# Attention and two MLP layers in float32: a new instruction order over 16 blocks, and weight preparation moved into attention

## What is computed

```python
# attention: 12288 queries, kv (384, 32, 128) pooled 4x4 to 768 keys
kv_pool = kv.reshape(B, H // r, r, W // r, r, C).mean(axis=(2, 4))
k = v = kv_pool.reshape(B, -1, C) @ w_sr
s = scale * (q @ k.transpose(0, 2, 1)); s = s - s.max(-1, keepdims=True)
a = np.exp(s); a /= a.sum(-1, keepdims=True) + 1e-09
x = a @ v
# layer 1
h = x @ w_in
x = (np.maximum(h, 0.0) + alpha * np.minimum(h, 0.0)) @ w_out
# layer 2
h = x @ w_in2; h2 = h * h; h3 = h2 * h
P = a[0] + a[1] * h + a[2] * h2 + a[3] * h3
Q = 1.0 + np.abs(b[0]) * np.abs(h) + np.abs(b[1]) * h2
out = (P / (Q + 1e-06)) @ w_out2
```

## Time and profile before

| | us |
|---|---|
| median of 3 runs (lowest, highest) | 1619.42 (1613.58, 1620.19) |
| the profiled execution's own time | 1616.42 |
| its span, first to last instruction | 1614.3 |

### The profile page before, as it was taken

How to read it: one execution, slowest core, us unless ns; L and a number is a source line. 1 busy time by engine, 2 the same in 40 slices (tenths; PEclk the granted TensorE clock), 3 DMA queues, 4 the chain that set the end, 5 groups by cost and what they waited for, 6 DMA issues and landing times. The chain is left out here.

```text
span 1614.3 us, 22125 instructions
## 1 busy us (share of the span) xinstructions
PE 1555.7 (96%) x5869; PEld 1015.0 (63%) x5869; DVE 1412.7 (88%) x2175; ACT 1398.8 (87%) x2659; POOL 1149.2 (71%) x1256
## 2 busy tenths in 40 slices
PE   6899999989999999999999999999999999999976
PEld 5799999845566565655565555656656555656532
DVE  3688888727999999999999999999999999999997
ACT  2577777628999999999999999999999999999996
POOL 0344444306888888888888888888888888888887
PEclk9999999999999999999999999999999999999998
DMA  8110100000000000000000000000000000000000
...
DMA packets 12299, 24.54 MB, mean 15 GB/s; under 512 B 1536, under 2 KB 1680, under 8 KB 11920
## 3 DMA queue, kind: packets, MB, share of 16 engines
...
q10 hardware_dynamic: 752, 0.60, 0.1%
...
## 5 line engine op out<-in xcount | busy, mean ns | idle before, releaser
L256 POOL TENSOR_TENSOR cubic<-sq,lin_p 128x512 f32<-128x512 f32 x384 | 492.4, 1283 | 225.4 <-ACT lin_p L408 178.0
L659 PE MATMUL banks<-x_hi,win_lo 128*128 128x512 f32 x768 | 508.4, 662 | 25.2 <-DVE ratio L591 15.3
L248 POOL TENSOR_TENSOR rational<-newton,ratio 128x512 f32<-128x512 f32 x288 | 368.6, 1280 | 35.8 <-PE banks L829 13.6
L818 PE MATMUL banks<-neg_part,wout 128*128 128x512 f32 x768 | 388.0, 593 | 0.3 <-ACT neg_part L386 0.3
L829 PE MATMUL banks<-rational,wout 128*128 128x512 f32 x768 | 379.2, 601 | 4.2 <-POOL rational L248 4.1
L577 DVE SCALAR_TENSOR_TENSOR banks<-sq,abs_b,banks 128x512 f32<-128x512 f32 x384 | 282.3, 752 | 59.2 <-ACT banks L402 57.2
L661 PE MATMUL banks<-x_hi,win_hi 128*128 128x512 f32 x768 | 303.7, 395 | 0.0
L660 PE MATMUL banks<-x_lo,win_hi 128*128 128x512 f32 x768 | 303.3, 395 | 0.0
L591 DVE SCALAR_TENSOR_TENSOR ratio<-banks,ab_raw,rcp 128x512 f32<-128x512 f32 x384 | 285.5, 743 | 1.3 <-ACT rcp L422 1.2
L583 DVE SCALAR_TENSOR_TENSOR banks<-banks,ab_raw,cubic 128x512 f32<-128x512 f32 x384 | 280.0, 752 | 0.0
L659 PEld LDWEIGHTS banks<-x_hi,win_lo 128*128 128x128 f32 x768 | 145.1, 189 | 205.1 <-issue 67.7
...
## 6 DMA issues: line engine op xcount, KB each, us to landing
...
```

The source lines that it names most:

```text
L248: nc.gpsimd.tensor_tensor(rational[:, m % 3, :], newton[:, m % 2, :], ratio[:, m % 2, :], ALU.mult).then_inc(s["rat_done"], 1)
L256: nc.gpsimd.tensor_tensor(cubic[:, m % 2, :], sq[:, m % 2, :], lin_p[:, m % 2, :], ALU.mult).then_inc(s["cubic_done"], 1)
L659: nc.tensor.matmul(dst, w[1], x[0], start=start, stop=False)
L818: nc.tensor.matmul(banks[:, ACC1, :], wout1[:, c, :], neg_part[:, n % 2, :], start=False, stop=(c == BLOCKS - 1)).then_inc(s["m1_done"], 1)
```

## The change

Layers: the pattern of four blocks gives way to one order of 16 blocks, written out for each engine, with layer 2 following 18 blocks behind. The win1 parts are negated, so that the negative part is a plain Relu. For the eight odd blocks the negative part is split (`neg_hi` by ScalarE, `neg_lo` by VectorE) and `out1` makes three float32r passes with a split w_out1. Of the others VectorE makes the negative part of block 14 alone; it keeps the finals of blocks 4 and 12 instead of four. `out2` makes four products of 128 columns with the data as weights, so that ACC2 comes out with the tokens in the partitions; the copy and the transposes of the output are gone. `negative` waits for `m1_done` of n - 3 instead of n - 1.

Load and attention: kv is loaded first. w_in1 is turned in step 0, the linear weight made in step 1, w_in1 split in steps 4 to 7 and w_in2 in steps 10 to 13 in pieces of 512 columns, w_out1 scaled in steps 16 to 19. The queries of group g + 1 are turned in step g, those of group 1 in the load phase. After the last step w_out1's odd blocks are split, and TensorE's first hidden product waits for that.

The diff, cut to its core:

```diff
-QUAD = 4
-DEPTH = 5 * QUAD
-BY_DVE_FINAL, BY_DVE_RELU = 2, 3
+BY_DVE_FINAL, BY_DVE_RELU = (4, 12), (14,)
+SPLIT = (1, 3, 5, 7, 9, 11, 13, 15)
...
+        wout1_hi, wout1_lo = sb("wout1_hi", [P, len(SPLIT), P], F32R), sb("wout1_lo", [P, len(SPLIT), P], F32R)
+        neg_hi, neg_lo = sb("neg_hi", [P, 2, GROUP], F32R), sb("neg_lo", [P, 2, GROUP], F32R)
...
+        IN1_STEP, IN2_STEP, SCALE_STEP, OUT2_STEP = 4, 10, 16, 15
+        PIECES = 4
...
-            sp.dma_start(raw_in[0], w_in1).then_inc(s["ld_in1"], 16)
             for c in range(CHUNKS):
-                if c == 3:
-                    sp.dma_start(wout1[:], w_out1.rearrange("(b p) c -> p b c", p=P)).then_inc(s["ld_out1"], 16)
-            sp.wait_ge(s["v_lo_done"], 2)
-            sp.dma_start(raw_in[1], w_in2).then_inc(s["ld_in2"], 16)
-            with sp.Fori(0, GROUPS // 2 - 1) as pair:
-                for u in (0, 1):
-                    sp.wait_ge(s["qt_ready"], pair * 2 + (1 + u))
-                    sp.dma_start(q_in[:, u, :], q_groups[pair * 2 + (2 + u)]).then_inc(s[f"ld_q{u}"], 16)
-
-            sp.wait_ge(s["in2_lo_done"], 1)
-            sp.dma_start(wout2[:], w_out2.rearrange("(b p) c -> p b c", p=P)).then_inc(s["ld_out2"], 16)
+            sp.dma_start(raw_in[0], w_in1).then_inc(s["ld_in1"], 16)
+            sp.dma_start(wout1[:], w_out1.rearrange("(b p) c -> p b c", p=P)).then_inc(s["ld_out1"], 16)
+            for g in range(GROUPS - 2):
+                sp.wait_ge(s["qt_ready"], g + 1)
+                sp.dma_start(q_in[:, g % 2, :], q_groups[g + 2]).then_inc(s[f"ld_q{g % 2}"], 16)
+                if g == 2:
+                    sp.wait_ge(s["v_lo_done"], 2)
+                    sp.dma_start(raw_in[1], w_in2).then_inc(s["ld_in2"], 16)
+                if g == OUT2_STEP:
+                    sp.wait_ge(s["in2_lo_done"], PIECES)
+                    sp.dma_start(wout2[:], w_out2.rearrange("(b p) c -> p b c", p=P)).then_inc(s["ld_out2"], 16)
             with sp.Fori(0, GROUPS) as g:
...
         @block.gpsimd
...
+            for p in range(GROUPS + 2):
+                final(p - 2, 14)
+                correction(p - 2, 15)
+                cubic_term(p - 1, 1)
+                final(p - 2, 15)
...
+                correction(p - 1, 14)
+                cubic_term(p, 0)
 
...
         @block.scalar
...
+                nc.scalar.activation(hi[:, piece(k)], raw[:, piece(k)], ACT.Copy, scale=-1.0 if name == "in1" else 1.0).then_inc(s[f"{name}_hi_done"], 1)
 
             act.wait_ge(s["ld_ab"], 32)
...
-            in1_transposed()
             copy_pooled_t(0)
             query_hi(0)
-            weight_hi(raw_in[0], win1_hi, "in1")
             copy_pooled_t(1)
-            act.wait_ge(s["lin_ready"], 1)
-            nc.scalar.activation(lin_hi[:], banks[:, 1, 0:P], ACT.Copy).then_inc(s["lin_hi_done"], 1)
+            query_hi(1)
             copy_pooled_t(2)
             copy_pooled_t(3)
...
                 exps(g, 0)
                 probs_hi(g - 2, 5)
                 exps(g, 1)
+                if g == 0:
+                    in1_transposed(0)
+                    in1_transposed(1)
+                if g == 1:
+                    linear_hi()
                 probs_hi(g - 1, 0)
                 attended_hi(g - 2)
                 probs_hi(g - 1, 1)
                 exps(g, 2)
-            weight_hi(raw_in[1], win2_hi, "in2")
+                if g == 0:
+                    in1_transposed(2)
+                    in1_transposed(3)
+                if IN1_STEP <= g < IN1_STEP + PIECES:
+                    weight_hi(raw_in[0], win1_hi, "in1", g - IN1_STEP)
+                if IN2_STEP <= g < IN2_STEP + PIECES:
+                    weight_hi(raw_in[1], win2_hi, "in2", g - IN2_STEP)
+            act.wait_ge(s["out1_scaled"], PIECES)
+            act.wait_ge(s["s_ready"], GROUPS * TILES)
+            nc.scalar.activation(wout1_hi[:], wout1_odd, ACT.Copy).then_inc(s["out1_hi_done"], 1)
 
 
...
+                    after(act, s["m1_done"], n - 3)
+                    kept = neg_hi if c in SPLIT else neg_part
+                    nc.scalar.activation(kept[:, c // 2 % 2, :], banks[:, H1, :], ACT.Relu).then_inc(s["neg_done"], 1)
...
+            for p in range(GROUPS + 3):
+                scaled_abs(p - 3, 14)
+                hidden_hi(p - 2)
+                square(p - 3, 15)
+                scaled_abs(p - 3, 15)
+                linear_part(p - 3, 15)
+                log(p - 3, 14)
+                negative(p - 1, 1)
+                inverse_q(p - 3, 14)
+                log(p - 3, 15)
+                linear_part(p - 2, 0)
+                square(p - 2, 0)
+                inverse_q(p - 3, 15)
+                scaled_abs(p - 2, 0)
+                negative(p - 1, 2)
...
+                inverse_q(p - 2, 13)
+                negative(p, 0)
...
         @block.vector
...
                 dve.wait_ge(s[f"ld_{name}"], 16)
-                dve.wait_ge(s[f"{name}_hi_done"], 1)
-                nc.vector.tensor_tensor(lo[:], raw, hi[:].bitcast(F32), ALU.subtract).then_inc(s[f"{name}_lo_done"], 1)
+                dve.wait_ge(s[f"{name}_hi_done"], k + 1)
+                nc.vector.scalar_tensor_tensor(lo[:, piece(k)], raw[:, piece(k)], -1.0 if name == "in1" else 1.0,
+                                               hi[:, piece(k)].bitcast(F32), ALU.mult, ALU.subtract).then_inc(s[f"{name}_lo_done"], 1)
...
+            def scale_out1(k):
...
-            weight_lo(raw_in[0], win1_hi, win1_lo, "in1")
+            query_lo(1)
             pool_keys(3)
-            dve.wait_ge(s["lin_hi_done"], 1)
-            nc.vector.tensor_tensor(lin_lo[:], banks[:, 1, 0:P], lin_hi[:].bitcast(F32),
-                                    ALU.subtract).then_inc(s["lin_lo_done"], 1)
             pool_keys(4)
             keys_lo(0)
             pool_keys(5)
+            values_lo(0)
             keys_lo(1)
-            values_lo(0)
-            values_lo(1)
             for g in range(STEPS):
                 if g > 0:
-                    query_lo(g)
+                    query_lo(g + 1)
                 probs_lo(g - 2, 2)
...
+                if SCALE_STEP <= g < SCALE_STEP + PIECES:
+                    scale_out1(g - SCALE_STEP)
+            dve.wait_ge(s["out1_hi_done"], 1)
+            nc.vector.tensor_tensor(wout1_lo[:], wout1_odd, wout1_hi[:].bitcast(F32), ALU.subtract).then_inc(s["out1_lo_done"], 1)
...
+            def negative_lo(g, c):
+                if group(g):
+                    dve.wait_ge(s["neg_done"], made(g, c, BY_ACT_RELU))
+                    nc.vector.scalar_tensor_tensor(neg_lo[:, c // 2 % 2, :], banks[:, H1, :], 0.0,
+                                                   neg_hi[:, c // 2 % 2, :].bitcast(F32),
+                                                   ALU.max, ALU.subtract).then_inc(s["neg_lo_done"], 1)
...
+                    nc.vector.tensor_scalar(y_out[:], banks[:, ACC2, :], -1.0, None, ALU.mult).then_inc(s["y2_out_done"], 1)
...
+            for p in range(GROUPS + 3):
+                place_output(p - 3)
+                denominator(p - 2, 3)
+                polynomial(p - 2, 2)
+                negative_lo(p - 1, 5)
+                check_product(p - 2, 2)
+                quotient(p - 2, 2)
+                check_product(p - 2, 3)
+                polynomial(p - 2, 3)
+                denominator(p - 2, 4)
+                quotient(p - 2, 3)
+                denominator(p - 2, 5)
+                polynomial(p - 2, 4)
+                negative_lo(p - 1, 7)
+                quotient(p - 2, 4)
+                check_product(p - 2, 4)
...
         @block.tensor
...
+            def linear_weight(first, end):
...
             pe.wait_ge(s["k_lo_done"], 2)
-            pe.wait_ge(s["v_lo_done"], 2)
             for g in range(STEPS):
                 if g > 0:
-                    queries(g)
+                    queries(g + 1)
                 weighted(g - 2, 0)
                 weighted(g - 2, 1)
                 transposed(g - 2, 3)
                 tile_scores(g, 0)
+                if g == 1:
+                    linear_weight(0, 6)
                 transposed(g - 2, 4)
                 weighted(g - 2, 2)
                 tile_scores(g, 1)
+                if g == 0:
+                    turn_in1(0)
+                    turn_in1(1)
+                if g == 1:
+                    linear_weight(6, 11)
                 weighted(g - 2, 3)
                 transposed(g - 2, 5)
                 weighted(g - 2, 4)
                 tile_scores(g, 2)
+                if g == 1:
+                    linear_weight(11, BLOCKS)
                 transposed(g - 1, 0)
                 weighted(g - 2, 5)
                 transposed(g - 1, 1)
                 tile_scores(g, 3)
+                if g == 0:
+                    turn_in1(2)
+                    turn_in1(3)
                 transposed(g - 1, 2)
 
 
-            for name in ("in1_lo_done", "lin_lo_done", "out1_scaled"):
-                pe.wait_ge(s[name], 1)
```

(65 more changed lines are left out.)

583 lines of the change are left out of this document (355 added, 228 removed).

## The result

| | before | after |
|---|---|---|
| median of the runs | 1618.54 us (4 runs, 1613.58 to 1620.19) | 1562.49 us (4 runs, 1560.67 to 1564.52) |
| ratio, 95% interval | | 0.9659 [0.9634, 0.9684] |
| profiled execution, its span | 1616.4, 1614.3 | 1564.5, 1562.7 |

A forecast was written before the change was run, and what follows sets the result against it. TensorE was taken to bound the kernel before and after. Layers -11.8 us and load and attention -4.6 gave -16.4, from 1616.4 to 1600 us, with a range of 1578 to 1619.

The forecast's parts named there:

- the seam's 3.1 us: Between attention and layers: TensorE's first hidden product waits for the split of wout1, +3.1 us.
- For stall I take the 0.8 of today: Steady layers: TensorE's stall per group stays 0.8 us, so its sum of 50.3 becomes a pace of 51.1.
- rival C: Layers: the new order has no stalls, 50.3 us per group, 1582 us in all; chance 0.17.
- the output product by 128 columns: Second layer on TensorE: four products of 128 columns cost 0.93 us for 0.856, +1.2 per group.
- the drain: Last 18 blocks of layer 2: paced by GpSimd's 47.1 us per group, 53.0 us, a gain of 0.6.
- Slack is at least 0.5 us everywhere: H1 bank in the layers: hidden products have at least 0.5 us of room, so their wait costs nothing.
- A: Layers: queueing among TensorE, VectorE and ScalarE eats the gain, pace stays 51.6 us per group, 1612 us; chance 0.22.
- B: Layers: GpSimd becomes the bound and the kernel slower, up to 1678 us, deciding from 0.25 us per cubic; chance 0.12.
- D: Second-layer output products: loading data as weights is not hidden, +400 us, 2000 us in all; chance 0.01.
- E: Load phase: no gain, because the pooling chain and not transfers limits it, +8 us, 1608; chance 0.04.
- The load phase: Start to first scores: 9.0 us less, of which 8.0 from moving w_in1 and w_out1 behind kv.
- The lead: Layer-1 blocks before the first layer-2 product: 18 blocks in 36.7 us for 40.5, a gain of 3.8.

The follow-up runs named there:

- both_light: Kernel after, leaving out ten float32r passes per group on TensorE and making `neg_lo` over 128 of 512 columns only: 1556.7 us, 49.35 per group.
- no_split: Kernel after without the split: odd blocks' negatives stay one float32 product, no `neg_lo`, no split of `wout1`: 1585.7 us, 50.93 per group.
- quad_out2: att_only plus the second-layer output product as four of 128 columns, in the old order of four blocks: 1604.6 us, 51.57 per group.
- att_only: Load and attention phases of the kernel after with the layers of the kernel before: 1612.7 us, for 1617.7 of the kernel before beside it.
- late_lo: Kernel after with each of the eight `negative_lo` one position later in VectorE's list: 1641.8 us, 52.99 per group.
- early_lo: Kernel after with each of the eight `negative_lo` one position earlier in VectorE's list: 1596.9 us, 51.14 per group.
- hold: Kernel after, with SyncE waiting for kv chunk 4 before it issues the w_in1 and w_out1 transfers: 1561.5 us.
- seam edit: Kernel after with the split of `wout1` moved to the end of step 24 of the attention: 1560.2 us.

## Why the prediction was wrong

**Right.** TensorE bound the kernel before, and the chance of 0.73 stood on faster. The split was priced at -1.3 per group and is worth 1.26. VectorE's 49.1 by starts was near: it is full at 49.6, and two finals more cost 1.10. ScalarE's need, 50.4 less 1.4, held as well (full at 49.35 in both_light). Load and attention gave 3.6 at the first hidden product, for 4.6; the seam's 3.1 us came as 3.09.

**The step that failed** is "For stall I take the 0.8 of today". With the measured price of the output products, TensorE's sum for a group after is 120 float32r passes (27.8), 8 float32 products (6.85), the linear term (0.7) and 16 x 0.89 (14.2): 49.6, and the pace is 49.67. In no_split the sum is 96 x 0.232 + 16 x 0.856 + 0.7 + 14.2 = 50.9 for a measured 50.93. In the order of 16 blocks TensorE runs at its bare sum; in the order of four it stands 0.7 (quad_out2, 51.57 for 50.9) to 0.8 us above it (att_only, 51.64 for 50.8). The stall went with what the change replaced, so it could not be carried over; that it was the order, and not the three negatives moved or ScalarE's looser wait, is likely but was not separated. The prediction held a piece of the evidence: I traced the stall to the H1 waits of the old order and priced the new order's slack there, but drew no conclusion for the stall. I also read one of three rows: beside the 28.5 us for ScalarE's negative part stood 26.5 for VectorE's and 26.1 for `ratio`. Together they are 3.8 us per group and not 0.8, because a weight load that waits is not yet a TensorE that stands. That the stall would go was rival C, to which I gave 0.17.

**A mis-sized term** put even rival C too high: the output product by 128 columns, taken as 0.93 from the pooling products, is 0.89 (0.111 per record for 0.116), 0.6 us per group. The two together are 1.4 per group, 51.1 for 49.67, or 366 x (3.192 - 3.104) = 32 of the 37 us. The other 5 are the drain, which I laid at GpSimd's full 47.1 / 16 = 2.95 per block and which took 2.67. For the -0.07 of quad_out2 the price explains +0.1; the other 0.2 may be a little stall that went with this edit already, and what took it was not tried. One slip changes nothing: the profiled 1616.4 lies 1.3 below the mean of the three times, not 1.0.

**Right for the wrong reason.** "Slack is at least 0.5 us everywhere, so I price this wait at nothing": nothing was lost, but late_lo loses 0.42 us per odd block from a delay of 0.6. By these two numbers the slack is about 0.2 us, an estimate. The step counted a chain that starts when the hidden product ends, as if VectorE were free at that moment; how much of the missing 0.3 us its list takes was not measured.

**The rivals.** A (queueing eats the gain) did not come, though its premise did: three full engines, and the hidden products' waits fell from 81.1 to 29.3 us. late_lo and early_lo show how near it was: eight instructions moved by one place give 52.99 and 51.14 per group. B fell with 0.08 us ahead of a cubic for the 0.25 from which it decides. D fell: 128-column records start 0.111 apart though each has a weight load of its own. The Trainium skill (TensorE: Matmul & The Clock Gate, Part 3) lets a weight load overlap running matmuls where the row group differs or where it goes into the background weight buffer. The row group is the same here (128x128 each time) and the loads are hidden all the same, so D did not follow from that rule; whether the background buffer is what hides them, no row shows. E fell too: the load part gained.

**The load phase** gave 6.1 of 9.0. About 1 us of what is missing is that the weight transfers, moved behind kv in the queue, still shared the DMA engines with the last chunk (hold); the rest is open. The lead gave 2.4 of 3.8, and the seam edit shows that the slow clock behind the idle stretch took 1.8 us there.
